# Routing digits of the next expert placed earlier, and ahead of the output transposes, in a fused attention and expert kernel

## The reference

```python
# 1. attention, q k v of (4, 8, 576, 64): pooled attention over groups of 4 positions, repeated,
#    plus local attention over |i - j| < 4
out = repeat(sm_attn(q_d, k_d, v_d), 4) + sm_attn_masked(q, k, v)      # -> x of (2304, 512)
# 2. dense layer: h = x @ w_in (512, 2048); g = piecewise square of h; x = g @ w_out
# 3. experts: N = 2304 tokens, E = 8 experts, cap = N // E = 288 tokens each
logits = x @ w_gate                                   # (2304, 8)
order = argsort(-logits.flatten())
for idx in order:                                     # best pairs first
    tok, e = idx // E, idx % E
    if assigned[tok] >= 0 or counts[e] >= cap: continue
    assigned[tok] = e; counts[e] += 1
for e in range(E):
    out[assigned == e] = relu(x[assigned == e] @ w1[e]) @ w2[e]       # w1 512x1024, w2 1024x512
```

## Time and profile before

| | us |
|---|---|
| median of 3 runs | 873.06 |
| lowest, highest | 872.46, 873.38 |
| the profiled execution: its time | 873.38 |
| the profiled execution: its span | 871.6 |
| round 0 of the experts (first step at 602.25) to round 1 | 35.6 |
| rounds 1 to 5, each | 32.9 to 33.0 |
| round 6 | 34 |

### The profile page before, as it was taken

One profiled execution on the slowest core, in us unless ns is written; L12 is line 12 of the kernel. 1 busy time (PEld: TensorE's weight loads), 2 busy tenths in 40 slices (PEclk: granted clock), 3 DMA queues, 4 the chain that ended last, 5 costly groups with the idle time before them and its releaser, 6 DMA issues. The chain is left out here.

```text
span 871.6 us, 21161 instructions
## 1 busy us (share of the span) xinstructions
PE 825.1 (95%) x7658; PEld 749.6 (86%) x7658; DVE 508.0 (58%) x1424; ACT 406.6 (47%) x1006; POOL 333.4 (38%) x391
## 2 busy tenths in 40 slices
PE   6979999999999999999999999939999999999995
PEld 5867888888889888888898989838999999999995
DVE  4667766655665665563534344366766766766620
ACT  4655555444535544553444444303454455455461
POOL 6661133203302321340000000007687786787882
PEclk8899999999999999999999999967999999999998
DMA  9975421320321233201101000006625625616611
GB/s 203 251 191 143 142 68 41 96 80 21 86 80 45 68 87 80 66 2 39 49 2 49 0 24 1 13 13 221 212 62 197 228 58 207 228 47 219 219 39 45
DMA packets 99301, 85.49 MB, mean 98 GB/s; under 512 B 63664, under 2 KB 71856, under 8 KB 99248
## 3 DMA queue, kind: packets, MB, share of 16 engines
q1 hardware_dynamic: 93808, 74.74, 29.5%
q0 software_dynamic: 3072, 9.44, 3.7%
q10 hardware_dynamic: 2368, 0.59, 0.4%
HBM read 70.60 MB, written 14.16 MB: 97 GB/s over the span
## 5 line engine op out<-in xcount | busy, mean ns | idle before, releaser
L528 PE MATMUL PS<-xs,W 128*128 128x256 f32 x1728 | 234.0, 285 | 1.3 <-DVE xT L432 1.3
L528 PEld LDWEIGHTS PS<-xs,W 128*128 128x128 f32 x1728 | 222.5, 189 | 12.4 <-issue 3.3
L528 PE MATMUL PS<-W,g 128*128 128x512 f32 x864 | 223.9, 396 | 5.4 <-DVE g L669 5.0
L528 PEld LDWEIGHTS PS<-W,g 128*128 128x128 f32 x864 | 152.4, 188 | 37.4 <-DVE g L669 9.6
L633 ACT ACTIVATE scratch<-PS,minus 128x256 f32<-128x256 f32 x144 | 68.3, 474 | 218.4 <-DVE scratch L660 218.4
L660 DVE TENSOR_SCALAR scratch<-PS 128x256 f32<-128x256 f32 x144 | 60.9, 423 | 124.9 <-PE PS L528 124.4
L441 POOL TENSOR_TENSOR P<-P,top 128x640 f32<-128x640 f32 x11 | 13.9, 1262 | 224.4 <-DVE top L391 224.4
L1539 POOL TENSOR_TENSOR w1s<-w1r,w1s 128x512 fp32r<-128x512 f32 x64 | 80.9, 1291 | 29.1 <-ACT w1s L1427 28.8
L1334 PE MATMUL PS<-exs,w1s 128*128 128x288 f32 x256 | 81.1, 317 | 0.0
L1334 PE MATMUL PS<-ehs,w2s 128*128 128x288 f32 x256 | 80.9, 316 | 0.0
L1335 PE MATMUL PS<-exs,w1s 128*128 128x288 f32 x256 | 76.1, 297 | 0.0
(11 more groups left out here) (198 smaller groups left out, 1449.8 us busy)
## 6 DMA issues: line engine op xcount, KB each, us to landing
w1r<-in_moe_w SPq DMA_DIRECT2D x16, 1024.0 KB, 5.0
w2r<-in_moe_w SPq DMA_DIRECT2D x16, 1024.0 KB
vd<-in_v SPq DMA_DIRECT2D x16, 288.0 KB
xt<-xT SPq DMA_DIRECT2D x16, 288.0 KB, 2.2
y<-scratch SPq DMA_DIRECT2D x18, 256.0 KB, 2.1
vw<-in_v SPq DMA_DIRECT2D x34, 128.0 KB, 2.8
scratch<-in_moe_w_in SPq DMA_DIRECT2D x8, 512.0 KB, 6.1
scratch<-in_moe_w_out SPq DMA_DIRECT2D x8, 512.0 KB, 5.4
```

Of the source, the lines that this page charges most:

```text
L528: r = pe.matmul(psum, wsel(w[i]), xsel(x[j]), start=first and t == 0, stop=last and t == 2)
```

## The change

The last digit's count and sum come one step earlier (after steps 18 and 19, not 19 and 20); in round 0 the last two digits do (14, 15 and 20, 21, not 15, 16 and 21, 22). And within a step `pe_round` issues counts and sums ahead of the y turns, not behind them. VectorE's code is not edited, but its order follows the lists: at step 19 the pick of the last digit now comes ahead of the split of hidden tile 4, and `dve_ahead` ahead of that of tile 5; in round 0 the pick of digit 4 comes ahead of the split of tile 3. Counts and turns share a step at 3, 49 and 55.

```diff
--- before.py
+++ after.py
@@ -1311,10 +1311,10 @@
 
         STEPS1, STEPS2 = EFC * KC, KC * EFC
 
-        COUNT = [49, 55, 61, 3, 10, 19]
-        SUM = [51, 58, 63, 5, 13, 20]
-        COUNT_FIRST = [0, 0, 4, 9, 15, 21]
-        SUM_FIRST = [0, 0, 5, 10, 16, 22]
+        COUNT = [49, 55, 61, 3, 10, 18]
+        SUM = [51, 58, 63, 5, 13, 19]
+        COUNT_FIRST = [0, 0, 4, 9, 14, 20]
+        SUM_FIRST = [0, 0, 5, 10, 15, 21]
         RANK, LIST = 28, 40
         TURN_X = [59, 59, 62, 62]
         TURN_X_LAST = [61, 61, 62, 62]
@@ -1405,14 +1405,14 @@
                               f == 0, f == EFC - 1)
                     if f == EFC - 1:
                         x.then_inc(ey_ready, 1)
+                for m, i in digits_at(s, r, COUNT, COUNT_FIRST, first, following, second):
+                    pe_count(pe, m, i)
+                for m, i in digits_at(s, r, SUM, SUM_FIRST, first, following, second):
+                    pe_sum(pe, m, i)
                 if not first and s == TURN_LAST:
                     pe_turn_y(pe, r - 1, KC - 1)
                 if s in TURN_Y:
                     pe_turn_y(pe, r, TURN_Y.index(s))
-                for m, i in digits_at(s, r, COUNT, COUNT_FIRST, first, following, second):
-                    pe_count(pe, m, i)
-                for m, i in digits_at(s, r, SUM, SUM_FIRST, first, following, second):
-                    pe_sum(pe, m, i)
                 if following and s == RANK:
                     pe_rank(pe, r + 1)
                 if following and s == LIST:
```

## The result

The changed kernel took 877.80 us (median of 7, 875.68 to 880.44) beside 873.15 us for the kernel before on the same chip (median of 7): ratio 1.0058, interval 1.0039 to 1.0077. It is 0.6% slower. The forecast of 875.2 had the sign and half of the size; the time lies above the range. The profiled execution took 878.07 us (span 876.4).

The account below looks back on a forecast made before the run. TensorE, busy 95% of the span, was taken as the bound. 1.5 + 0.1 + 0.24 + 0.27 = 2.1 us on the median of 873.06 gave 875.2 us, 0.24% slower; range 873.4 to 876.7, forecast's chance 0.66.

Parts of the forecast that it names:

- the order at step 3: Rounds 1 to 6: the count still waits for `over`, the y turn comes behind it; +0.25 us a round, 1.5 in all.
- steps 49 and 55: Count ahead of y turn: +0.25 and -0.08, together +0.17 us a round, mostly taken by the gather's wait; 0.1 left.
- The wait at step 18: Last count one step earlier, just behind the end of `over`: waits 0.04 us a round, 0.24 in six rounds.
- rival (b): Earlier choice brings the gather forward, so waits at step 59 go: 1.7 us faster, 871.4 us; chance 0.04.
- (a): Rival: only the saved switch counts, 0.08 at each of 18 meetings; 1.4 us faster, 871.6 us; chance 0.05.
- (d): Rival: wait at step 3 half hidden by weight loading, step 18 free; 1.1 us slower, 874.2 us; chance 0.17.
- Sum and count stay one step apart, so `full` has the same time: Steps 18 and 19: moving the last count and sum together leaves the time for `full` unchanged; no cost put on it.
- I cost it at nothing: Delayed y turns reach ScalarE 0.5 to 0.8 us later, but it waits there anyway and GpSimd's weights have slack; zero.
- Rival (c): Late turn tiles at ScalarE make the x tiles late: 0.4 us more in five rounds, 877.2 us; chance 0.08.
- Round 0: Count at step 14 waits for `over`, step 15 comes 0.40 later; +0.27 us reaches the gather, bounds 0 and 0.48.

Follow-up runs that it names:

- e3: The changed kernel with GpSimd's third scatter issued one piece of weights later; 876.12 us, 1.0018 of the kernel before.
- e13: The changed kernel, unedited, as a control in a later session; 875.97 us beside 873.34 for the kernel before, 1.0022.
- marker: The changed kernel plus a small ScalarE copy that waits for the last count's signal, ahead of hidden tile 4's relu; 878.11 us beside 875.30, one run each.
- e1: The kernel before with only the order within a step changed, lists of steps as before; 875.53 us beside 873.90, 1.0012.
- e5: The changed kernel with the y turn of step 3 back ahead of the count; 874.74 us beside 873.84 for the kernel before, 1.0014.
- e14: The changed kernel, unedited, repeated in a further session; 875.69 us beside 873.43 for the kernel before, 1.0027.
- e4: The kernel before with only GpSimd's third scatter one piece of weights later, over the last count; 878.95 us, 1.0054.
- e6: The changed kernel with its last sum back at step 20, the count at 18; 877.79 us, 1.0032 of the kernel before.
- e15: The same kernel as e4, unedited, in another session; 873.29 us, 0.9996 of the kernel before.
- e16: The kernel before with the first two x turns at step 60, not 59, repeated unedited; 870.53 us, 0.9963.

## Why the prediction was off

**Right: the price of the order at step 3.** Predicted +0.25 a round; the sum of step 5 stands 3.56 into the round and not 3.35, +0.21, 1.3 us in six rounds. Count at `over`'s end plus 0.06, as read from the earlier trace rows.

**Right: steps 49 and 55, and where their cost goes.** Predicted +0.17 a round, taken by the gather's wait but for 0.1 us in all. Measured: from the rank matmul (step 28) to the sum of step 58 14.67 became 14.86, +0.19 a round; on to the x turn of step 59, the mean of rounds 1 to 5 went from 15.37 to 15.39, 0.1 us in five. The x turn of round 1 now starts at 668.49, 0.17 after the last matmul at 668.32, where it took 0.27; in round 2 it starts 0.13 after. The Trainium skill (TensorE: Matmul & The Clock Gate, Part 2, Step-by-step: what each phase is for) has weight loads pulled ahead of matmuls in flight. At step 55 the new order saved 0.06, where that rule, as the forecast read it, gave nothing; how much such a pull hides around groups this small, no run here shows.

**The wait at step 18, and the rivals.** A wait of 0.04 was predicted; the count starts without one. Nothing was gained by the earlier choice, so rival (b) fell; (a) and (d) fell with the full 0.21 at step 3.

**Missed, small: the sum ahead of a new tile.** "Sum and count stay one step apart, so `full` has the same time" is true, but the sum itself now stands ahead of step 20, and what follows it starts 0.18 later and not 0.04: +0.14 a round. Without a wait of the sum it is less, 0.09 in e3 and e13 (681.83 to 681.92 above): +0.05.

**Failed: "I cost it at nothing".** This is the sentence on the delayed turns, that they hand their tile to ScalarE later and that ScalarE waits there anyway. ScalarE does. Behind its copy, though, stands GpSimd's first scatter, and behind that, in GpSimd's strict order, two more and the weights. I looked at the weights and not at the scatters. They came 0.66 later; the third reached the count of the last digit, and where the hold is, the mark was late by 0.58. The sum had 0.09 to spare, so +0.49 a round. Rival (c) had the delay but the wrong victim, the x tiles.

**Round 0.** Predicted +0.27, from the 0.40 at step 14. The stall is there (idle 0.32 at 611.79, answer to the earlier trace rows) and the round is 35.58 beside 35.59. But up to the sum of step 10, ahead of every step that the change moves, the two traces already differ (10.26 us before, 10.09 changed), and from that sum to the x turn of step 59 the changed kernel takes 21.87 and not 21.71: +0.16. Over the experiments with the x turns at step 59 and no marker in round 0, this stretch took 21.61 to 22.50 with either list, so a term of 0.16 or 0.27 can't be told from chance. The granted clock adds to it: it was 0.50 (1.2 GHz) from 603.13 to 605.90 in e1, and 1.00 (2.4 GHz) from 602.40 on in e5; the round took 35.68 there and 34.47 here, and 33.67 to 36.71 over all experiments.

```profile
611.79 0.59 PE L1286 MATMUL PS<-hot,over 128*128 128x8 bf16 x18 [0.32 <-DVE over L1137]
```

**The sum made again.** In rounds 1 to 5: 0.21 for the order, 0.49 for the hold, 0.14 behind the sum, together 0.84, and the rank matmul stands 14.84 into the round and not 13.99; 0.02 more by the x turns: 0.86, against 0.79 to 0.92 measured (mean 0.84). Round 6: 0.7 later at the rank matmul (14.79 into the round, not 14.10), and its wait for the gather of 0.61, which stood at 832.54 in the kernel before, is gone: +0.12 in the end. Without the hold the same list gives 0.21 + 0.05 = 0.26, and the rank matmul of e13 stands at 14.27, +0.27. With longer waits for the gather in some rounds, e13 and e14 have +1.94 and +1.81 in rounds 1 to 6, and ratios of 1.0022 and 1.0027, 1.9 and 2.4 us of 873. The forecast was 2.1. That these agree is in part luck: the 0.24 of step 18 and the 0.27 of round 0 were not found, and what was found behind the sum and in the waits for the gather was not in it. The size of the first result was missed by the term that was put at zero.

**How far the cause is shown.** That the scatter over the count makes the loss in the sessions with the hold is shown: e3 takes it out of the changed kernel by moving the scatter, e5 most of it by moving the turn, and e4 makes it in the kernel before by nothing else. Why the mark is late is open, but the kept traces narrow it: VectorE is not held alone. The marker ran only in sessions without a hold, yet ScalarE has waits of its own for signals that TensorE gives behind a count. The changed kernel, round 2:

```profile
682.47 0.29 PE L1336 MATMUL PS<-exs,w1s 128*128 128x288 f32 x1
682.87 0.16 DVE L1184 TENSOR_SCALAR full<-PS 64x8 bf16<-64x8 f32 x1 [0.91 <-PE PS L1286]
682.92 0.41 ACT L1461 ACTIVATE ehs<-PS 128x288 fp32r<-128x288 f32 x1 [1.34 <-PE PS L1336]
```

The relu of hidden tile 4 starts 0.45 after the start of the matmul of step 19 that it waits for, and 0.05 after the late mark. In e13 it starts 0.33 after it (681.70 to 682.03 above) and 0.50 after the mark. So it is in rounds 1 to 5 of both profiles of the changed kernel with the hold (0.42 to 0.47, always 0.05 after the mark). At step 55 it is the same: ScalarE's copy `yo` waits for the turn behind the count and starts 0.55 after it in every round of e13 and e14, but 0.55 to 0.64 after it in e1, e3, e5 and e6, 0.04 to 0.06 after the late mark each time. What these waits have in common is a signal of TensorE. A count's signal that is late or arrives late, with TensorE's next signals behind it, fits; where it is held up, no run tells.

The Trainium skill (SBUF — State Buffer, Who interferes with whom) has VectorE and GpSimd take turns on a shared pair of ports for whole instructions. A `tensor_scalar` can take the pair only where its operands meet conditions, a `tensor_reduce` never does on trn2, and an instruction with at most one input in SBUF stays clear of it outside the two-port modes. That doesn't explain the hold: the mark is a `tensor_scalar` that reads PSUM (`full<-PS`), and nothing here shows it in such a mode; ScalarE is held with it; the mark starts 0.41 to 0.47 after the row of the scatter has ended, not at its end; and in three sessions the same overlap holds nothing (e13, e15). The pick, a reduce, is not held under a scatter, as the page has it: at 679.76, under the second scatter of the changed kernel's round 2 (679.05 to 679.98), it stands 7.65 into the round, as in e13.

Nor is every wait for TensorE held. The timeline of the changed kernel, round 2, under its first scatter (676.63 to 677.57, shown above):

```profile
676.46 0.29 PE L1336 MATMUL PS<-exs,w1s 128*128 128x288 f32 x1
...
676.79 0.41 ACT L1461 ACTIVATE ehs<-PS 128x288 fp32r<-128x288 f32 x1 [0.63 <-PE PS L1336]
```

ScalarE's relu starts 0.33 after the start of the matmul that it waits for, inside the scatter, and 0.34 after it at step 3, outside one (673.64 to 673.98). What differs between the sessions, no run tells.

## What to carry to other kernels

When an instruction moves later on an engine that never idles, follow its result through every engine behind it until something has slack, with each queue's fixed order: here TensorE's turn, ScalarE's copy, three scatters on GpSimd, and a VectorE mark eight microseconds later. Give a wait its cover before shortening the chain ahead of it: moving the x turns a step later gained 0.2 to 0.4%, where the earlier digits and the new order lost 0.2 to 0.6%. When halves of an edit don't add up to the whole, look for two things that have begun to meet; and repeat a sub-percent result in another session before giving it one number.

## What the runs showed of the hardware

An idle VectorE starts a small instruction 0.64 us after the start of the count whose signal it waits for; under the issue row of an indirect DMA of GpSimd (0.93 us) it started at 1.22 in the changed kernel and at 1.55 in e4, in three sessions, and at 0.64 in three others, with the same kernels. A ScalarE instruction that waits for TensorE's next signal behind the count was late with it, 0.05 after VectorE's (0.45 and not 0.33 after its matmul). The mark of step 55, whose count starts under a gather, shows it too: 0.90 to 0.93 in the kernel before and 0.98 to 1.04 in the two profiles of the changed one, but 0.63 to 0.65 in e13 and e16. So one and the same change cost 0.58% and 0.55% in two sessions, and 0.22% and 0.27% in two others.
